# Attention head pairs: own and left-hand scores folded into one square from the third query tile on, and the keys' high part moved to ScalarE

## What is computed

```python
# q, k, v: (2, 8, 768, 64); n_sink = 4, window = 128
scores = scale * q @ k.T
keep = (pos_k < n_sink) | ((rel >= 0) & (rel < window))   # rel = pos_q - pos_k
a = softmax(where(keep, scores, -1e9))
x = (a @ v), heads side by side
h = relu(x @ w_in); u, v = halves of h
x = (u * (w_spatial @ normalise(v) + b_spatial)) @ w_out
u = x + w_tok2.T @ relu(w_tok1.T @ x); out = u + relu(u @ w_ch1) @ w_ch2
```

## Time and profile before

| what | us |
|---|---|
| median of 3 runs (509.27 to 510.44) | 509.32 |
| the profiled execution | 509.37 |
| its span, first to last instruction | 507.5 |
| PE busy | 492.1 |
| DVE busy | 211.1 |
| POOL busy | 171.0 |
| ACT busy | 163.5 |

### The profile page before, as it was taken

The page is one execution under the profiler, slowest core; times in us unless marked ns, Lnnn a source line. Parts: engine busy times, 40 slices in busy tenths (PEclk is TensorE's granted clock), DMA queues, the critical chain, the costliest instruction groups (busy, mean ns, idle before and its releaser), DMA issues.

```text
span 507.5 us, 7154 instructions
## 1 busy us (share of the span) xinstructions
PE 492.1 (97%) x2664; PEld 436.1 (86%) x2664; DVE 211.1 (42%) x527; ACT 163.5 (32%) x343; POOL 171.0 (34%) x185
## 2 busy tenths in 40 slices
PE   3899999999999999999999999999999999999997
PEld 2788989999999899999888898888888888888885
DVE  5577777677676416754222232112131131211212
ACT  5577656565556242112342232010010010010010
POOL 3655653654451488701305057970000000000000
PEclk9999999999999999999999999999999999999999
DMA  7455322432311134300202013420020000100002
GB/s 238 150 166 170 112 77 86 137 118 91 106 43 33 61 96 134 89 0 1 77 1 65 19 45 102 136 72 0 1 83 1 0 1 0 70 14 0 1 0 83
DMA packets 19189, 34.03 MB, mean 67 GB/s; under 512 B 2256, under 2 KB 4560, under 8 KB 19152
## 3 DMA queue, kind: packets, MB, share of 16 engines
q1 hardware_dynamic: 19008, 33.55, 21.1%
q10 hardware_dynamic: 144, 0.00, 0.0%
HBM read 30.39 MB, written 3.15 MB: 66 GB/s over the span
## 4 chain that ended last, share of the span: by engine, by line
PE 89%; POOL 4%; DMA 2%; DVE 2%; issue 2%; ACT 1%; SPq 0%; ACTq 0%; POOLq 0%; DVEq 0%
PE bank L950 24%; PE bank L951 24%; PE bank L952 24%; PE bank L1023 6%; PE bank L989 3%; PE bank L965 2%; PE bank L966 2%; PE bank L1031 1%; PE bank L1182 1%; PE bank L1005 1%; POOL win_lo L539 1%; POOL k_lo L517 1%; DMA stage<-w_in 1%; DMA stage<-w_sp 1%; POOL wsp_lo L539 1%
## 5 line engine op out<-in xcount | busy, mean ns | idle before, releaser
L939 DVE SCALAR_TENSOR_TENSOR hch_lo<-bank,hch_hi 128x512 fp32r<-128x512 f32 x36 | 24.9, 692 | 153.8 <-ACT hch_hi L728 153.8
L728 ACT ACTIVATE hch_hi<-bank 128x512 fp32r<-128x512 f32 x36 | 21.5, 598 | 169.0 <-PE bank L952 169.0
L611 ACT ACTIVATE probs<-masked,small 128x288 f32<-128x288 f32 (+1 forms) x96 | 49.0, 512 | 49.5 <-DVE small L780 49.2
L780 DVE CUSTOM_DVE_ANT_0 masked<-bank,masks 128x288 f32<-128x288 f32 (+1 forms) x96 | 41.0, 428 | 38.9 <-PE bank L966 33.8
L952 PE MATMUL bank<-up_hi,wc_lo 128*128 128x512 f32 x144 | 56.0, 389 | 0.0
L951 PE MATMUL bank<-up_lo,wc_hi 128*128 128x512 f32 x144 | 56.0, 389 | 0.0
L950 PE MATMUL bank<-hch_hi,wc_hi 128*128 128x512 f32 x144 | 56.0, 389 | 0.0
L951 PE MATMUL bank<-hch_lo,wc_hi 128*128 128x512 f32 x144 | 56.0, 389 | 0.0
L950 PE MATMUL bank<-up_hi,wc_hi 128*128 128x512 f32 x144 | 56.0, 389 | 0.0
L952 PE MATMUL bank<-hch_hi,wc_lo 128*128 128x512 f32 x144 | 56.0, 389 | 0.0
L1023 PE MATMUL bank<-v_sl,p_t 128*128 128x66 f32 x352 | 46.8, 276 | 0.0
(11 more groups left out here) (121 smaller groups left out, 1022.7 us busy)
## 6 DMA issues: line engine op xcount, KB each, us to landing
k_raw<-kT SPq DMA_DIRECT2D x24, 256.0 KB, 3.1
q_raw<-qT SPq DMA_DIRECT2D x24, 256.0 KB, 2.9
stage<-w_c SPq DMA_DIRECT2D x24, 256.0 KB, 2.7
v_sl<-vL SPq DMA_DIRECT2D x12, 264.0 KB, 2.9
outT<-out_sb SPq DMA_DIRECT2D x12, 256.0 KB, 2.1
stage<-w_sp SPq DMA_DIRECT2D x12, 192.0 KB, 2.5
stage<-w_in SPq DMA_DIRECT2D x8, 256.0 KB, 3.6
stage<-w_out SPq DMA_DIRECT2D x4, 256.0 KB, 3.2
```

The lines of the kernel that those rows point to most:

```text
L611: act.activation(probs[:, n % N_PROB, 0:w], masked[:, n % N_MASKED, 0:w], ACT.Exp, bias=least[:, n % 8:n % 8 + 1], scale=-1.0).then_inc(ex ...
L728: act.activation(hch_hi[:, u[2] % N_HCH, :], bank[:, :], ACT.Relu).then_inc(hi_ready, 1)
L780: dve.tensor_tensor_reduce(masked[:, n % N_MASKED, 0:w], score_bank[n % 2][:, 0:w], masks[:, m:m + w], 1.0, 3e38, ALU.add, ALU.min, least[ ...
L939: dve.scalar_tensor_tensor(out=hch_lo[:, f % N_HCH, :], in0=bank[:, :], scalar=0.0, in1=hch_hi[:, f % N_HCH, :], op0=ALU.max, op1=ALU.subt ...
```

## The change

For tiles with i at least 2 (8 of 12, 64 heads, 32 pairs), PE's scores stay as they were. DVE then copies, in the score bank, the own keys' scores over the left-hand keys' scores where the query isn't before the key (`copy_predicated`, 128x128, with a triangle of ones `tri_own` as predicate), and signals itself. Mask, exponential and turning then take 160 and 128 columns instead of 288 and 256: one square a head. The values are P times V_left plus (P, own triangle alone) times (V_own - V_left). So ACT copies the turned pair as it is (256 columns), DVE writes it once more, multiplied by a triangle, into the other half of `p_t` (256 columns), and POOL computes V_own - V_left (`value_difference`, two halves a tile, 16 in all). PE's `values` has four matmuls a pair as before. ACT's `pair_out` waits for DVE's where there is one.

With i = 1 (2 tiles) the score product now leaves the sinks out (256 columns), and ACT and DVE copy half a pair each; with i = 0 ACT copies each pair (256 columns) alone. The keys' high part (22 of POOL's instructions) becomes an ACT instruction behind `exps` and `sinks_gather` at n % 4 = 0. One later mask less is made.

```diff
@@ k_prepare, POOL @@
-                if g >= 2:
-                    pool.wait_ge(s_k[g % 2], 16 * (g // 2 + 1))
-                    if g >= 4:
-                        pool.wait_ge(scored, 4 * (g - 1))
-                    pool.tensor_scalar(k_hi[:, hs, c0:c0 + P], raw, 1.0, 1.0, ALU.mult, ALU.mult).then_inc(k_high_done, 1)
                 pool.wait_ge(k_high_done, g + 1)
                 pool.tensor_tensor(k_lo[:, hs, c0:c0 + P], raw, k_hi[:, hs, c0:c0 + P], ALU.subtract).then_inc(k_ready, 1)
+            def value_difference(t, half):
+                cols = slice(GV * half, GV * half + GV)
...
+                pool.wait_ge(valued, 4 * (t - 1) + 2 * half + 2)
+                pool.tensor_tensor(v_diff[:, cols], v_sl[:, t % 3, cols], v_sl[:, (t - 1) % 3, cols], ALU.subtract)\
+                    .then_inc(diff_ready, 1)
@@ the loop over n, POOL @@
+                if n % 4 == 1 and (n // 8, n % 8 // 4) in diff_n:
+                    value_difference(n // 8, n % 8 // 4)
@@ ACT @@
             def pair_out(m):
                 act.wait_ge(turned, turn_index[("pair", m)] + 1)
+                if m in halved_n:
+                    act.wait_ge(pt_dve, halved_n[m])
...
-                for m in range(0, N_PAIR, 2):
+                for m in range(N_PAIR):
                     if turn_step(m) == n:
                         pair_out(m)
...
+                if n % 4 == 0 and 2 <= n // 4 + 1 < N_GROUP:
+                    k_high(n // 4 + 1)
@@ mask_scores, DVE @@
                 dve.wait_ge(scored, n + 1)
+                if merged(t):
+                    own, previous = (odd, even) if t % 2 else (even, odd)
+                    dve.copy_predicated(previous, tri_own.bitcast(U32), own).then_inc(own_placed, 1)
                 if n >= N_MASKED:
                     dve.wait_ge(exped, n - N_MASKED + 1)
+                if merged(t):
+                    dve.wait_ge(own_placed, placed_n[n])
@@ pair_out, DVE @@
-                dve.tensor_copy(p_t[:, m % N_PT, 0:cols], tr_bank[turn_index[("pair", m)] % 2][:, 0:cols]).then_inc(pt_dve, 1)
+                if merged(m // 4):
+                    dve.tensor_tensor(half.rearrange("p (h c) -> p h c", c=P), bank[:, 0:2 * P].rearrange("p (h c) -> p h c", c=P),
+                                      tri_turned.unsqueeze(1).to_broadcast([P, 2, P]), ALU.mult).then_inc(pt_dve, 1)
+                else:
+                    dve.tensor_copy(half, bank[:, 2 * P:4 * P]).then_inc(pt_dve, 1)
...
-                for m in range(1, N_PAIR, 2):
+                for m in HALVED:
                     if turn_step(m) == n:
                         pair_out(m)
@@ turn_pair, PE @@
-                    for c, _ in blocks(m // 4):
+                    for c in squares(m // 4):
@@ values, PE @@
+                    else:
+                        parts = [(P * n, v_sl[:, (t - 1) % 3, :]), (2 * P + P * n, v_diff)]
```

More of the change, by code:

```diff
@@ L128, with merged, in_bank, in_slot @@
 sink_n = {g: n for n, g in enumerate(SINK_GROUPS)}
[L130 to L135, removed]
+MASK_FIRST, MASK_SECOND, MASK_SQUARE = 0, P, 3 * P
+TRI_OWN, TRI_TURNED = 4 * P + 2 * SINKS, 5 * P + 2 * SINKS
+MASK_COLS = 6 * P + 2 * SINKS
+SLOT = 2 * P
+def merged(t):
+    return t % NT >= 2
+def in_bank(t):
+    i = t % NT
+    return slice(0, P) if i == 0 else slice(0, SLOT) if i == 1 else slice(0, P + SINKS) if i % 2 else slice(P, BAND)
+def in_slot(t):
+    i = t % NT
+    return slice(0, P) if i == 0 else slice(0, SLOT) if i == 1 else slice(0, P + SINKS) if i % 2 else slice(P - SINKS, SLOT)
+def sinks_in_slot(t):
+    return slice(P, P + SINKS) if t % 2 else slice(P - SINKS, P)
 def mask_at(t):
     i = t % NT
-    return MASK_FIRST if i == 0 else MASK_SECOND if i == 1 else MASK_ODD if i % 2 else MASK_EVEN
-def blocks(t):
+    return MASK_FIRST if i == 0 else MASK_SECOND if i == 1 else MASK_SQUARE + SINKS if i % 2 else MASK_SQUARE
+def squares(t):
     i = t % NT
-    own = (0 if i % 2 == 0 else P + SINKS, t % 3)
-    return [own] if i == 0 else [(P + SINKS if i % 2 == 0 else 0, (t - 1) % 3), own]
+    return [0] if i == 0 else [0, P] if i == 1 else [0] if i % 2 else [P]
+HALVED = [m for m in range(N_PAIR) if m // 4 % NT]
+halved_n = {m: n + 1 for n, m in enumerate(HALVED)}
+DIFFS = [(t, half) for t in range(TILES) if merged(t) for half in range(2)]
+diff_n = {d: n + 1 for n, d in enumerate(DIFFS)}
+placed_n = {n: 1 + sum(merged(e // H) for e in range(n)) for n in range(N_HEAD)}
 A_K_HI, A_K_LO = 0, 8 * BAND
@@ L175 @@
 COLS = E_ID + P
-assert all(at % P == 0 for at in (A_V, A_PROBS, A_PT, A_PTS, A_CAT, A_X, B_X, X_SLOT, B_WIN, C_VN, D_U, E_V, E_STAGE, E_ID))
+assert H * DV <= 5 * P
+assert all(at % P == 0 for at in (A_V, A_DIFF, A_PROBS, A_PT, A_PTS, A_CAT, A_X, B_X, X_SLOT, B_WIN, C_VN, D_U, E_V, E_STAGE, E_ID))
 A_WSP = 0
@@ L227, in build @@
         scratch = at("mask_scratch", B_X + X_SLOT, [8, P])
-        rel_sb, key_sb, diag_keep, prev_keep, sink_keep, first_keep, second_keep = (scratch[:, i, :] for i in range(7))
+        rel_sb, key_sb, diag_keep, prev_keep, sink_keep, first_keep, second_keep, square_keep = (scratch[:, i, :] for i in range(8))
+        tri_own, tri_turned = masks[:, TRI_OWN:TRI_OWN + P], masks[:, TRI_TURNED:TRI_TURNED + P]
         x_hi = [at(f"x_hi{i}", B_X + X_SLOT * i, [KT, HALF], F32R) for i in range(2)]
@@ L602, in exps @@
             def exps(n):
[L603 to L604 removed]
+                cols = in_slot(n // H)
                 act.wait_ge(masked_ready, n + 1)
@@ L1014, in values @@
                     pe.wait_ge(x_nat_ready, g - 1)
-                if m % 2 == 0:
-                    pe.wait_ge(pt_act, m // 2 + 1)
-                else:
-                    pe.wait_ge(pt_dve, m // 2 + 1)
-                at_ = 0
-                for head in (2 * m, 2 * m + 1):
-                    h, place = head % H, head % 4
-                    for _, slot in blocks(t):
+                pe.wait_ge(pt_act, m + 1)
+                if m in halved_n:
+                    pe.wait_ge(pt_dve, halved_n[m])
+                if (t, g % 2) in diff_n and m % 2 == 0:
+                    pe.wait_ge(diff_ready, diff_n[t, g % 2])
+                first = m % 2 == 0
+                for n in range(2):
+                    h, place = (2 * m + n) % H, (2 * m + n) % 4
+                    if t % NT == 0:
+                        parts = [(P * n, v_sl[:, t % 3, :])]
+                    elif t % NT == 1:
+                        parts = [(2 * P * n, v_sl[:, (t - 1) % 3, :]), (2 * P * n + P, v_sl[:, t % 3, :])]
+                    else:
+                        parts = [(P * n, v_sl[:, (t - 1) % 3, :]), (2 * P + P * n, v_diff)]
+                    for at_, v in parts:
                         ins = pe.matmul(bank[:, DV * place:DV * place + DV], p_t[:, m % N_PT, at_:at_ + P],
-                                        v_sl[:, slot, DV * h:DV * h + DV], start=m % 2 == 0 and at_ == 0, stop=False,
-                                        skip_group_check=True)
-                        at_ += P
+                                        v[:, DV * h:DV * h + DV], start=first, stop=False, skip_group_check=True)
+                        first = False
                 if ("sink", g) in turn_index and m % 2:
```

85 lines of the change are left out of this document (51 added, 34 removed).

## The result

| | before | after |
|---|---|---|
| median, us | 509.88 (4 runs, 509.27 to 510.88) | 521.53 (4 runs, 521.2 to 521.9) |
| ratio | | 1.0227 [1.0206, 1.0248] |
| profiled execution, its span | 509.37, 507.5 | 521.90, 520.1 |

The forecast was 511.4 us, with 506 to 517 as the range. The direction was right and the size wasn't: 11.7 us lost instead of 2, outside the range.

What follows compares the result with a forecast made beforehand. PE's own work was taken to bound the attention steps. From 509.37 us, 7.2 saved and waits of 4.6, 2.1 and 2.7 added gave 511.6, said as 511.4 with 0.2 from the start; 8-in-10 range 506.0 to 517.0.

Steps and rivals of the forecast that it cites:

- What bounds the kernel, and where room matters: Attention steps: PE's own work bounds, busy 135.3 of 136.0 us; little room at sink turns and turns of x.
- What is removed, 7.2 us: PE: 32 pairs lose two squares each, 6.9 us; narrower scores in tiles with i = 1 give 0.3.
- one that waits begins 0.04 after it: DVE: the mask waiting for the copy's signal begins 0.04 us after the copy's end; a head costs 0.19 more.
- A: Sink turn in a tile's second step: PE waits for DVE's longer chain, 4.6 us over seven tiles.
- B: Sink turn in a tile's sixth step: 0.14 us each in five of eight, 2.1 us in all.
- C: Turn of x directly behind the sixth step's sink turn: PE waits 0.45 us in six tiles, 2.7 us.
- ACT gets 22 high parts ... all of it is hidden: ACT: 22 keys' high parts, at most 0.74 us each, leave it below 100 of 136 us; hidden on average.
- POOL "nothing": POOL: 22 instructions given for 16, with 36.1 us of waiting in the line that goes, so no cost.
- Rival 1: DVE: the copy's wait for its signal costs nothing; 506.5 us, or 504.5 with a copy of 0.23; chance 0.27.
- Rival 2: DVE: the predicated copy takes 0.46 us, 518.5 us; each 0.1 us of copy costs 4.1; chance 0.13.
- Rival 3: Keys come late to PE behind ACT's exponential and gathering: 519 us; chance 0.05, shared with PE's clock falling.
- Rival 4: PE's waits at sink turns and turns of x overlap: 509.5 to 510.5 us, no difference; chance 0.2.

Runs made afterwards that it cites:

- run 3: Changed kernel with the sink turn and the turn of x each one step later, no instruction more or less: 510.04 us, 1.0004.
- run 4: Kernel before with the sink turn and the turn of x each one step later: 508.72 us, 0.9977.
- run 13: Changed kernel with both turns one step later, keys' high part back on POOL, and no predicated copy or its signal: 502.97 us, 0.9873.
- Run 2: Kernel before with only the keys' high part moved to ACT: 509.35 us, 0.9988.
- run 1: Changed kernel with the keys' high part moved back from ACT to POOL, 22 instructions: 519.44 us, 1.0194.
- run 6: Changed kernel without POOL's differences of the values, the own values used instead: 516.55 us, 1.0136.
- run 10: Changed kernel with a plain copy of 128 columns in place of the predicated one: 520.19 us in one execution.

## Why the prediction was right in direction and wrong in size

- **What bounds the kernel, and where room matters.** Right. No other engine became full, and the time went to single turns where PE asks for what was made one step before. Moving the asking by one step gave 11.5 us back (run 3), and 1.3 in the kernel before (run 4).
- **What is removed, 7.2 us.** Right to 1.4 to 1.9 us (run 13 against run 4).
- **The copy 0.29, the mask 0.32.** Right (0.291, 0.325).
- **"one that waits begins 0.04 after it".** Wrong for this instruction: 0.14. The 0.04 was read from rows where a tile outside the banks is written. It makes the head +0.29 instead of +0.19. With that, A becomes 4.6 + 0.3 x 7 = 6.7, and 5.2 more than before were measured. That A came out near its forecast is in part luck: steps 73, 81 and 49 waited 0.4 us longer each, and step 33, forecast at 0.55, not at all, because the clock had just fallen. The rule of the Trainium skill (VectorE: DVE Perf Modes, The DRAIN you can't avoid), which would have made it +0.07, is the further off: the traces don't agree with it.
- **At B "the same head sum", 0.14 each.** This is the step that failed worst, 2.1 against 5.3. The 3.2 us between them have three main parts. The gap makes 0.10 in each place, 0.8. I charged the place with its own head alone, and took the DVE ahead of it as idle, as it was before (1.09 us of waiting ahead of head 68); in step 69 two dearer heads, a product and a wait for ACT used that up, for 0.5. The cover had to be counted through to the last idle time of DVE, not over one head. And I took the query instruction in that stretch as it was: ahead of steps 37 and 45 it took 1.78 and 1.76 us behind POOL's `vn_lo`, and these two turns take 1.9 over their forecast, 0.2 of it the gap.
- **C, 2.7.** Measured 2.3. The cause is as forecast, ACT's copy; the sum hit with some luck, since it came as seven waits, mostly of 0.3, one of them in step 29, and not as six of 0.45.
- **"ACT gets 22 high parts ... all of it is hidden".** Half wrong. Run 2 shows no cost in the kernel before, run 1 shows 2.1 us in the changed one, where the move changes what POOL runs as the queries begin. The queries' high part, behind ACT's pair copy, comes late to DVE (0.34 us at 120.00), and the query instruction is slower when POOL works beside it.
- **POOL "nothing".** Wrong as a sum of price and effect: 15 differences of 0.8 us, without which the kernel takes 5.0 us less (run 6). The price counted POOL's own time alone, and not what POOL's instructions do to DVE's.
- **Rivals.** Rival 1 is refuted by the gap of 0.14. Its 504.5 us, with a copy of 0.23, should have been 504.0 by the 4.1 us for each 0.1 of rival 2. Rival 2's condition, a slow copy, is false (0.291), but a head did come out 0.10 dearer, by the gap. By the rival's own 4.1 us for each 0.1 us that makes 515.5; A to C came out 3.4 over their forecast. Rival 3 is refuted as told: PE never waits for the keys' low part. The falling clock that stood beside it at 0.05 came in some of the executions, and those without it are as slow. Rival 4, the waits overlapping, didn't come as an answer: the time is 11.7 us over, not level. What it says of one wait shortening the next is seen once, at step 33.
- **Left out.** The later start of the product behind the sink turn (1.3), the clock (1.7, in this execution) and the stretch behind the last turn of x (1.5). That stretch took 336.7 to 336.9 us in the three versions of the kernel before, 337.5 to 338.6 in those of the changed kernel that have the copy, and 336.7 and 337.7 in the two without it. Why is open. Up to the first turn of x it is 25.8 to 28.0 us with no order by version, so the 0.6 in the ledger need not be of this change.

## What to carry to other kernels

When a change makes a helper engine's step longer, don't cost it at the place where it stands: walk back on that engine to its last idle time, add up everything new since then, and compare that with the idle time before charging anything to the waiter. If an engine's average is far from full and the waiter still waits, look first at where the waiter asks: one step of more distance was worth 11.5 us here. Count what runs on the neighbour engine at that moment too: one instruction that began 0.05 us behind POOL's took 1.1 us longer. And a helper that gets an instruction writing what its next one reads pays for the wait between them too.

## What the runs showed of the hardware

- On VectorE, an instruction that waits for the one before begins 0.14 to 0.15 us behind its end where that one wrote a bank (64 predicated copies, and the 64 plain ones of run 10), and 0.04 where it wrote elsewhere. The two kinds differ in the operation too.
- The query instruction takes 0.69 us alone. When it began while POOL ran an instruction of 128 x 256 elements or more, it ended 0.53 to 0.56 us behind that instruction's end, unless 0.69 us from its own start was later: 1.78 at 62.87 (`vn_lo` ended at 64.10), 1.10 at 127.61 (`v_diff` ended at 128.16). Of the 360 query instructions in the fifteen traces of these kernels 359 follow this to 0.03 us, and 99 took over 0.72; the one left began in the same 0.01 us as POOL's. One-column instructions of POOL don't count. It holds the other way too: `v_diff`, begun at 64.06 while that query instruction ran, took 1.21 instead of 0.75. In the kernel before the longest was 1.08. The Trainium skill (GPSIMD Engine Reference, section 1) says that the two engines share interfaces to SBUF and contend when DVE has two inputs there; the trace agrees, and gives it a size.
- PE can lose more than its wait: in the changed kernel the product with the values begins 0.23 to 0.24 us after a late sink turn, and 0.13 after the one that was on time. In the kernel before these are 0.14 to 0.15 and 0.10 to 0.11.
- After a wait of 1.32 us the granted clock fell to 0.50 for 3.4 us. After one of 1.29 at the same place in run 10 it didn't.
